# A linear attention followed by two mixture layers, fp32, one core: the first 32x32 inversions done in halves and joined on TensorE

## The reference, cut to what matters

```
q, k, v: (4, 8, 768, 48)   beta: (4, 8, 768)          # batch, heads, sequence, head size
k_n = k / (norm(k) + 1e-6)
for t in range(768):                                   # per batch and head, state is 48x48
    y[t] = q[t] @ state
    state = state + beta[t] * outer(k_n[t], v[t] - k_n[t] @ state)
x = y as rows (3072, 384)
x = silu(x @ w_in) @ w_out                             # w_in 384x2048, w_out 2048x384
# then: rows with x @ w_skip <= 0 pass unchanged; every other row takes the expert
# argmax(x @ w_gate) of 8:  x + gate * (relu(x @ w1[e]) @ w2[e])
```

## Time and profile before

| | |
|---|---|
| median of 3 runs | 820.12 us (819.48 to 822.68) |
| profiled execution, its own time | 824.12 us |
| its span, first to last instruction | 822.3 us |
| PE matmuls, weight loads, DVE, ACT, POOL busy | 95%, 87%, 69%, 44%, 14% of the span |
| mean granted TensorE clock | 0.989 |

### The profile page before, as it was taken

The page is one execution under the profiler, slowest core; times in us unless marked ns, Lnnn a source line. Parts: engine busy times, 40 slices in busy tenths (PEclk is TensorE's granted clock), DMA queues, the critical chain, the costliest instruction groups (busy, mean ns, idle before and its releaser), DMA issues.

```text
span 822.3 us, 28779 instructions
## 1 busy us (share of the span) xinstructions
PE 781.2 (95%) x12083; PEld 713.0 (87%) x12083; DVE 567.5 (69%) x1503; ACT 360.3 (44%) x1024; POOL 114.0 (14%) x287
## 2 busy tenths in 40 slices
PE   5877989999999999999999999999999999999993
PEld 3546878999989998899999999999999989999993
DVE  6969887877588775777867687654423577777751
ACT  3723433434435253453434535343443545656531
POOL 1000000001010010101002010010102153445542
PEclk9988999999999999999999999999999999999998
DMA  8772112121311223113130211211024447665610
GB/s 279 210 248 61 34 57 64 60 93 46 93 47 50 83 66 97 41 49 92 57 102 22 67 47 61 71 42 47 22 69 145 134 153 231 209 208 182 195 35 14
DMA packets 48094, 79.83 MB, mean 97 GB/s; under 512 B 5840, under 2 KB 35498, under 8 KB 47968
## 3 DMA queue, kind: packets, MB, share of 16 engines
q1 hardware_dynamic: 44544, 73.07, 27.7%
q0 software_dynamic: 3424, 4.93, 2.0%
HBM read 67.05 MB, written 13.19 MB: 98 GB/s over the span
## 4 chain that ended last, share of the span: by engine, by line
issue 73%; DMA 12%; POOL 8%; PE 3%; DVE 1%; POOLq 1%; ACT 0%; SPq 0%
DMA id_table<-token,slot 6%; DMA out<-kv_t,ids_all 5%; POOL idle L692 3%; PE psum L1003 2%; POOL id_table L737 2%; POOL out L773 1%; POOL kq_t L747 1%; DMA id_table<-x_sb 1%; POOL kq_t L799 1%; DMA x_sb<-kq 1%; PE psum L859 0%; PE psum L1004 0%; DMA ids_all<-id_table 0%; POOLq L769 0%; SPq L573 0%
## 5 line engine op out<-in xcount | busy, mean ns | idle before, releaser
L1037 PE MATMUL psum<-xt_hi,w_hi 128*128 128x256 f32 x768 | 225.1, 293 | 2.1 <-DVE xt_lo L1578 1.0
L1038 PE MATMUL psum<-xt_lo,w_hi 128*128 128x256 f32 x768 | 216.8, 282 | 0.0
L1039 PE MATMUL psum<-xt_hi,w_lo 128*128 128x256 f32 x768 | 216.6, 282 | 0.0
L1213 ACT ACTIVATE h_raw<-psum 128x256 f32<-128x256 f32 x192 | 73.7, 384 | 319.5 <-PE psum L1039 317.6
L1468 DVE TENSOR_TENSOR h_lo<-h_raw,h_hi 128x256 fp32r<-128x256 f32 x192 | 81.3, 423 | 156.5 <-ACT h_hi L1214 143.8
L1037 PEld LDWEIGHTS psum<-xt_hi,w_hi 128*128 128x128 f32 x768 | 144.5, 188 | 9.6 <-issue 2.2
L1039 PEld LDWEIGHTS psum<-xt_hi,w_lo 128*128 128x128 f32 x768 | 145.6, 190 | 0.0
L1038 PEld LDWEIGHTS psum<-xt_lo,w_hi 128*128 128x128 f32 x768 | 145.1, 189 | 0.0
L1061 PE MATMUL psum<-w_hi,h_hi 128*128 128x394 f32 x384 | 138.3, 360 | 0.8 <-DVE h_lo L1468 0.8
L1063 PE MATMUL psum<-w_hi,h_lo 128*128 128x394 f32 x384 | 131.2, 342 | 0.0
L1062 PE MATMUL psum<-w_lo,h_hi 128*128 128x394 f32 x384 | 131.0, 341 | 0.0
(11 more groups left out here) (187 smaller groups left out, 1094.6 us busy)
## 6 DMA issues: line engine op xcount, KB each, us to landing
kq_t<-kq SPq DMA_DIRECT2D x24, 512.0 KB, 3.5
bp<-moe_w SPq DMA_DIRECT2D x24, 512.0 KB, 5.3
kv_t<-kv SPq DMA_DIRECT2D x24, 384.0 KB, 3.2
bp<-moe_w SPq DMA_DIRECT2D x24, 384.0 KB, 4.6
kd<-kq SPq DMA_DIRECT2D x20, 256.0 KB
x_table<-x_sb SPq DMA_DIRECT2D x13, 392.0 KB, 3.0
out<-x_sb SPq DMA_DIRECT2D x12, 384.0 KB
bp<-moe_w_in SPq DMA_DIRECT2D x6, 512.0 KB, 6.3
```

Source lines behind the costliest of these rows:

```text
L1037: m(out, hi, x_hi, start=first, stop=False)
L1038: m(out, hi, x_lo, start=False, stop=False)
L1039: return m(out, lo, x_hi, start=False, stop=last)
L1213: a_.activation(h_raw[i % 2][:, :], up_ps[i % 2][:, 0:G2], ACT.Silu)
```

## The change

The first group's inversion is cut: `halves(k)`, k = 1 to 14, inverts both 16x16 halves of each block at once; `first_halves` transposes the first half's inverse and multiplies it by -gamma; after `turn_back(0)`, `across(v)` and `join(v)` (v = 0, 1; 64 matmuls each, 32x32 weights and 16 columns) make the quarter between the halves on PE, with DVE copying and adding. Groups 1 to 5 are inverted as before.

Stage buffers 0 and 1 and the rows' buffers now lie where `xt_hi`, `xt_lo`, `h_hi` and `h_lo` will be (`early_x`, `early_h`), `minus` has a place of its own. The key products and masks of step 1 stand before the pair loop's start without waiting for all pieces and rows; pieces 12 and 13, the three `rows` and the `scores` move into pair 0's slots; `warm` is gone. SP loads step 2's `kq` and `kv` right after the last piece.

```diff
-        xt_hi = [sb(f"xt_hi{i}", [P, KD, G2], F32R) for i in range(2)]
-        xt_lo = [sb(f"xt_lo{i}", [P, KD, G2], F32R) for i in range(2)]
+        with nc.sbuf_tensor("early_x", [P, 4 * KD * G2], F32) as early_x:
+            pass
+        xt_parts_of = [[sb(f"xt_{part}{i}", [P, KD, G2], F32R) for part in ("hi", "lo")] for i in range(2)]
...
+        with nc.sbuf_tensor("early_h", [P, 2 * RING * G2], F32) as early_h:
+            pass
...
-        minus = h_hi[:, 0, 0:P]
+        minus = sb("minus", [P, P], F32R)[:, :]
+        HALF = Q // 2
+        first_half = early_x[:, 2560:3072].rearrange("p (b c) -> p b c", c=HALF)
+        across = early_h[:, 1024:2048].rearrange("p (b c) -> p b c", c=Q)
...
-        stage = bp_half[2:6]
+        stage = [early_x[:, WCH * a:WCH * a + WCH] for a in range(2)] + bp_half[4:6]
...
-        SCORES_AT = {1: 0, 4: 1, 7: 2, 10: 3}
+        SCORES_AT = {28: 0, 29: 1, 30: 2, 31: 3}
+        WEIGHTS_AT = {4: 12, 7: 13}
+        ROWS_AT = {13: 0, 22: 1, 27: 2}
...
-        GRAM_AT = {7: (2, 0), 19: (2, 1), 25: (3, 0)}, {6: (2, 0), 12: (2, 1), 27: (3, 0), 30: (3, 1)}
+        GRAM_AT = {13: (2, 0), 19: (2, 1), 25: (3, 0)}, {6: (2, 0), 12: (2, 1), 27: (3, 0), 30: (3, 1)}
-        MASK_AT = {14: (2, 0), 20: (2, 1), 28: (3, 0), 34: (3, 1)}
+        MASK_AT = {16: (2, 0), 20: (2, 1), 28: (3, 0), 34: (3, 1)}
...
-            for k in range(1, Q - 1):
-                s["lanes"](0, k)
-                if k % 2 and 4 + k // 2 < WP:
-                    s["weights"](4 + k // 2)
-                if k in DIAG_AT:
-                    s["diag"](1, DIAG_AT.index(k))
-                if k == Q - 8:
-                    for e in range(2):
-                        s["evict"](1, 1, e)
-                if k == Q - 5:
-                    for a in range(2):
-                        s["gram"](1, a)
-                if k == Q - 3:
-                    for n in range(KD):
-                        s["rows"](n)
+            for k in range(1, HALF - 1):
+                s["halves"](k)
+            for n in range(4, 7):
+                s["weights"](n)
+            for n in range(2):
+                s["diag"](1, n)
+            s["weights"](7)
+            for n in range(2, 4):
+                s["diag"](1, n)
+            s["weights"](8)
+            s["first_halves"]()
             s["turn_back"](0)
+            for v in range(2):
+                s["across"](v)
+            s["weights"](9)
+            for e in range(2):
+                s["evict"](1, 1, e)
+            for v in range(2):
+                s["join"](v)
+            s["weights"](10)
             for a in range(2):
+                s["gram"](1, a)
                 s["mask"](1, a)
+            s["weights"](11)
...
-                    if p == 0 and x in (1, 2):
-                        s["warm"](5, WP)
+                    if p == 0 and x in WEIGHTS_AT:
+                        s["weights"](WEIGHTS_AT[x])
+                    if p == 0 and x in ROWS_AT:
+                        s["rows"](ROWS_AT[x])
...
             for i in range(8, WP):
                 load_weights(i)
+            load_kq(2)
+            load_kv(2)
...
-            for k in range(KD):
-                load_rows(k)
+            load_rows(0)
+            load_rows(1)
+            load_kq(3)
+            load_rows(2)
             sp.dma_start(id_table.rearrange("(p n) a -> p (n a)", p=P), nowhere).then_inc(table_blank, 16)
-            sp.wait_ge(rows_used, 1)
-            load_kq(2)
-            load_kv(2)
...
+            def across_part(v):
+                pe.wait_ge(halves_turned, 1)
+                if v == 0:
+                    pe.wait_ge(bp_ready, H)
+                for x in range(LN // 2 * v, LN // 2 * v + LN // 2):
+                    for q in range(TURN):
+                        rows, at = slice(Q * q, Q * q + Q), HALF * (x % (LN // 2))
+                        last = m(psum[rows, 6 + v, at:at + HALF], dg[rows, x, :], first_half[rows, x, :], start=True, stop=True)
+                last.then_inc(across_done, 1)
...
+            def join_part(v):
+                pe.wait_ge(blocks_turned, 1)
+                pe.wait_ge(across_out, v + 1)
...
+                        last = m(psum[rows, 6 + v, at:at + HALF], across[rows, x, :], xt_blk[rows, x, HALF:Q], start=True, stop=True)
+                last.then_inc(joined, 1)
...
+            d.memset(across[:, :, HALF:Q], 0.0)
...
-                    if t == 1:
-                        dve.wait_ge(w_rest, WP)
-                        dve.wait_ge(rows_used, KD)
...
+            def halves(k):
+                if k == 1:
+                    dve.wait_ge(inv_init, 1)
+                    d.memset(inv[:, :, :].rearrange("p i c -> p (i c)")[:, 0:Q * Q:Q + 1], 1.0)
+                    d.memset(inv[:, HALF:Q, 0:HALF], 0.0)
...
+                n = HALF - 1 - k
+                step = outer[:, 0:2 * n * k].rearrange("p (s i c) -> p s i c", s=2, c=k)
+                d.tensor_tensor(step, both(low, k + 1, n, k, -k), both(inv, k, -n, 0, k), ALU.mult).then_inc(lane_step, 1)
+                dve.wait_ge(lane_step, 2 * (k - 1) + 1)
+                of = both(inv, k + 1, n, 0, k)
+                d.tensor_tensor(of, of, step, ALU.add).then_inc(lane_step, 1)
```

More of the change, by code:

```diff
@@ L342, in lane_count, with both @@
         def lane_count(g, k):
-            return (2 * (Q - 2)) * g + 2 * (k - 1)
+            return (2 * (HALF - 2) + 2 * (Q - 2) * (g - 1) if g else 0) + 2 * (k - 1)
+        def both(x, row, rows, col, cols):
+            of, by_row, by_col = x[:, row:row + 1, col:col + 1], Q if rows > 0 else 0, 1 if cols > 0 else 0
+            return bass.AP(tensor=of.tensor, offset=of.offset, ap=[[Q * Q, P], [HALF * Q + HALF, 2], [by_row, abs(rows)], [by_col, abs(cols)]])
         LANE_SLOTS = range(41, 63), range(16, 58)
@@ L517, in steps @@
             names += ["mask", "diag", "evict", "squares", "norms", "spread", "begin", "scales", "gram", "turn", "lanes", "turn_back", "weights", "up", "lo", "down",
-                      "queries", "outputs", "rows", "scores", "first", "split", "x2", "choose", "rank", "place", "warm"]
+                      "queries", "outputs", "rows", "scores", "first", "split", "x2", "choose", "rank", "place", "halves", "first_halves", "across", "join"]
             assert set(given) <= set(names)
@@ L637, in _ @@
                 if t + 3 < T:
-                    load_kq(t + 3)
+                    if p:
+                        load_kq(t + 3)
                     load_kv(t + 3)
@@ L895, in gram @@
                 last.then_inc(gram_done, 1)
+            def across_part(v):
[10 more added lines that the diff above has]
+                pe.wait_ge(across_out, v + 1)
+                for x in range(LN // 2 * v, LN // 2 * v + LN // 2):
+                    for q in range(TURN):
+                        rows, at = slice(Q * q, Q * q + Q), LN // 2 * HALF + HALF * (x % (LN // 2))
+                        last = m(psum[rows, 6 + v, at:at + HALF], across[rows, x, :], xt_blk[rows, x, HALF:Q], start=True, stop=True)
+                last.then_inc(joined, 1)
             def r_free(t):
@@ L1005, in weights @@
                 last.then_inc(w_rest, 1)
-            def warm(n, weights_done):
-                pe.wait_ge(w_split, weights_done)
-                for _ in range(n):
-                    m(up_ps[1][:, 0:G2], w_hi[0][:, 0:P], w_hi[0][:, 0:G2], start=True, stop=True)
             def rows(k):
@@ L1107, in place @@
                     last.then_inc(xgt_ps[b], 1)
-            schedule(steps(first=first, place=place, diag=diag, gram=gram, read=read, solve=solve, carry=carry, update=update, outputs=outputs, weights=weights,
-                           queries=queries, up=up, down=down, rows=rows, scores=turn_scores, rank=rank_of, warm=warm))
+            schedule(steps(first=first, place=place, diag=diag, gram=gram, across=across_part, join=join_part, read=read, solve=solve, carry=carry, update=update, outputs=outputs, weights=weights,
+                           queries=queries, up=up, down=down, rows=rows, scores=turn_scores, rank=rank_of))
             def transposes(t, a):
@@ L1553, in split @@
                                 ALU.subtract).then_inc(ew_split, 1)
-            schedule(steps(first=first, split=lambda x: split(0, x, 0), evict=evict, squares=squares, norms=norms, scales=scales, spread=spread, mask=masked, turn=turn, lanes=lanes, turn_back=turn_back, read=read, carry=rest,
+            schedule(steps(first=first, split=lambda x: split(0, x, 0), evict=evict, squares=squares, norms=norms, scales=scales, spread=spread, mask=masked, halves=halves, first_halves=first_halves, across=across_part, join=join_part, turn=turn, lanes=lanes, turn_back=turn_back, read=read, carry=rest,
                            update=update, keep=keep, lo=lo, x2=x2, scores=split_scores, choose=choose, place=place))
```

56 lines of the change are left out of this document (39 added, 17 removed).

## The result

| | before | after |
|---|---|---|
| median of the runs | 819.8 us (819.27 to 822.68, 4 runs) | 833.73 us (831.39 to 834.26, 4 runs) |
| ratio, 95% interval | 1 | 1.0157 (1.0127 to 1.0188) |
| profiled execution, its own time | 824.12 us | 834.26 us |
| first `solve`, S | 61.50 | 62.66 |
| `up(0, 1)` | 81.44 | 94.10 |

The change costs 13.9 us by the medians, where 5.5 were forecast (825.6 us, range 817 to 833): slower as predicted, more than twice as much, and 0.7 us outside the range.

A forecast was written before the change was run, and what follows sets the result against it. PE bounds the kernel, so the change is worth what it moves `up(0, 1)`: S 61.4 plus pair 0's 25.5 gives 86.9, 5.5 us later; 820.12 + 5.5 = 825.6 us, range 817 to 833.

The forecast's parts named there:

- S: Start of pair 0's first `solve`, forecast at 61.4 us against 61.50 before, 9.6 us saved being spent on code waits.
- 1.4 us per 64 matmuls: Time on PE for each 64 matmuls of `across` and `join`, taken from `diag`'s 10.8 ns a record.
- The first edge: First code page edge PE meets in the burst before S: reached at 34.4, its page usable at 38.0 us.
- The five pages behind it: Five further code pages in PE's burst up to `join`, at 3.6 us each, 18.0 us in all.
- From there to S: After the last code page: rest of `join`, then piece 10, `gram` and piece 11 on PE, 5.4 us.
- The rival that code comes in time: Instruction buffer deep enough, no code waits before S: S at 51.9, 816.1 us; chance 0.13.
- S is where it was: Claim that the first `solve` stays put, 61.4 against the profiled 61.50, code waits using up the 9.6 us saved.
- Pair 0: Stretch from S to `up(0, 1)`: forecast 25.5 us against 19.9 before, terms summing to +5.6.
- The two pieces: Pieces 12 and 13 standing inside pair 0 on PE: +3.4 us.
- Rows and scores: In pair 0: `rows` +0.4 us; scores, behind other DVE work, delaying `up(0, 0)`: +2.5 us.
- The clock ahead of S: Clock term for pair 0: -0.7 us, for a clock that may hold better and score transposes moved out of the chain.
- The slow rival: Code pages before S at 4.6 us and the clock falling: S at 66.4, 833 us; chance 0.20.

The follow-up runs named there:

- e2_few: Changed kernel with only one lane in 16 of the `across` and `join` matmuls issued (part of the inverse then missing); 815.93 us, ratio 0.9960.
- e1_twice: Changed kernel with each matmul of `across` and `join` issued twice, same result; 849.29 us, ratio 1.0356.
- Second profile: Both kernels profiled again, unchanged, one run each: before 818.46 us (first `solve` 57.19), after 831.87 us (61.30).
- e3: Changed kernel with the thirty `lanes` steps for group 0 in place of `halves`, `across` and `join`; 825.90 us, ratio 1.0081.
- g4: e4 with rows and scores earlier in pair 0, and 30 matmuls of no use before the first `solve`; 815.20 us, ratio 0.9935.
- e4: e3 with pieces 12 and 13 before the pair loop as well; 822.57 us, ratio 1.0025.
- g2_spread: Changed kernel reordered on PE: `diag`s behind pieces 4 to 7, piece 8 between the `across`, piece 10 between the `join`; 832.30 us, ratio 1.0150.
- h1: Changed kernel in g2_spread's order, all pieces ahead of the pair, early rows and scores, 20 matmuls of no use before the pair; 833.90 us, ratio 1.0178.
- i2: The same kernel as h1, unchanged, run for another profile; 833.27 us (one run).

## Why the prediction was right in direction and too small

- **S.** Forecast 61.4, measured 62.66 and 61.30. DVE's times held (halves end 35.4 for 36.5, `first_halves` 37.3 for 38.2), as did 1.4 us per 64 matmuls (1.29 for 128 records without a stop). That the number is so close is in part luck, as three errors nearly cancel. The first edge, 114 records into the `diag` of 33.90, 127 before the stop at 38.83, was passed without a wait near 35.1 (114 x 10.3 ns behind 33.90), where I had 38.0: -2.9. The five pages behind it took 20.0 us to 55.05, 4.0 each and not 3.6: +2.0. From there to S it took 7.6 us, with 1.2 GHz for the first 5, and not 5.4: +2.2. I also had few transfers running while PE stands; beside the wait that ended at 55.05 they ran at 325 GB/s.
- **The rival that code comes in time** is out by `e2_few` and `e1_twice`. What the Trainium skill, "Runtime: NRT & Kernel Launch", Instruction fetch mechanics, says of a buffer of 2,048 instructions and crossings mostly hidden is not what these traces show: PE stands at every 127 or 128 records where the work between is short. What the same section says of the next page, that it is fetched while the current one runs, does agree with them. Nor does the Trainium skill's "TensorEngine Tiling (Array Packing)", Instruction Overhead, hold for these tiles: 10 ns a record where it gives some 25.
- **What S is compared with: the step that failed first.** "S is where it was" took 61.50 from the one profiled execution, and I took the whole sum over to the median by adding 5.5. But the 4.3 us by which that execution was slow lay in this very stretch, ahead of S, and the changed kernel no longer has the wait that made them. Second profile against second profile, the change makes S 4.1 us later, and this was counted as -0.1.
- **Pair 0: the step that failed second.** Forecast 25.5 us, measured 31.4 and 30.6, against 19.9 and 20.3 before: the +5.6 should have been +10.3 to +11.5. Taken together the terms are known: from `e3` to `g4` they come to 10.7 us, by the pair's length in the traces (30.85 to 20.12) and by the medians (825.90 to 815.20) alike. How they divide is less sure, as each trace is one execution. The two pieces are 5.4 us by the traces and 3.3 by the medians (I had 3.4; the profiled `e4` was 2.6 us below its median). Rows and scores are 4.0 and 3.6 (I had 2.9). The clock ahead of S is 1.4 and 3.8, of which the part behind `up(0, 1)` is not the clock's (I had -0.7). So the sign of the clock's term was wrong by either count, and rows and scores were somewhat under-priced; whether the pieces were is not settled. What I left out can be seen in the trace: after PE had stood for the scores' split, `up(0, 0)`, `gram` and `read` took 5.95 us at 1.2 GHz, where I had 3.4. The stop for code in the pair explains little, 2.05 and 2.46 us against 1.73 before.
- **Sum.** 4.1 + 10.3 = 14.4 between the two second profiles (818.46 and 831.87, 13.4 apart), against 13.9 between the medians. In these terms the forecast was -0.1 + 5.6.
- **The slow rival** (833, chance 0.20) had the right time for the wrong reason: it put the loss before S with pages of 4.6 us. The pages of the burst took 4.0, and the loss is mostly behind S.

Open: what sets the time of a page. From 42.48 to 46.20 it was 3.72 us beside 96 GB/s of transfers; the page that ended at 55.05 took some 4.1 beside 325, and the one of 5.93 us in `g2_spread` had 217. Open with it is why the spread order didn't help.

## What to carry to other kernels

A rewrite that saves one engine 12 us by several hundred tiny matmuls is priced in instructions: here 127 or 128 pairs of load and matmul in a burst cost 3.5 us or more, and twice the columns cost nothing that could be measured. When a base profile is slower than its median, ask in which stretch it is slow before taking a difference over: if the change rewrites that stretch, the slow part is not there to be kept. And a new wait of about 2 us on TensorE is to be priced with the clock that may fall behind it (2.6 us in one place here, nothing in another). Filling it with idle matmuls restored the clock in both places tried, and paid by the medians in one of them.

## What was not expected of the hardware

- 30 matmuls that compute nothing, in a stretch in which PE would have stood for 3.8 us, gave 3.8 us by the medians (815.20 against 819.02). The granted clock of the 20 us behind them rose from 0.93 to 1.00, and the `diag`s' waits for code behind `up(0, 1)` fell from 2.1 to 0.5 us.
- PE's waits for code differ between kernels far behind the edit: in the traces, up to 3 us of the differences between these kernels lie in `diag`s that no edit touched.
- Doubling the columns of 512 records from 16 to 32 did not slow them: 128 records in 1.31 us against 1.29, both at 2.4 GHz.
- Executions of one kernel differ by 4 us at `up(0, 1)` when the `rows` wait longer for a transfer (two cases: `rows(2)` in the kernel before, at 57.20 against 54.82, and in `h1` and `i2`, at 73.97 against 75.96), as the clock falls behind the longer wait.
